# Gathering, laying out and turning the later experts' rows without TensorE, a 32-column one-hot and bf16 compares in the first routing

## The reference

```python
# 1. retention attention: q, k, v are (4, 8, 768, 64)
for t in range(S):
    state = gamma * state + outer(k[t], v[t])
    y[t] = scale * q[t] @ state
x = y.transpose(0, 2, 1, 3).reshape(3072, 512)
# 2. mixture of experts with a capacity of cap = 3072 // 8 = 384 tokens each
logits = x @ w_gate                       # (3072, 8)
for idx in np.argsort(-logits.flatten()): # best (token, expert) pairs first
    tok, e = idx // 8, idx % 8
    if assigned[tok] >= 0 or counts[e] >= cap: continue
    assigned[tok] = e; counts[e] += 1
for e in range(8):
    mask = assigned == e
    out[mask] = np.maximum(x[mask] @ w1[e], 0) @ w2[e]     # 512 -> 1024 -> 512
# 3. gated layer, 512 -> 1536 -> 512
result = (sigmoid(out @ w_gate2) * (out @ w_val)) @ w_out
```

## Time and profile before

| | |
|---|---|
| time, median of 3 runs (lowest, highest) | 1104.27 us (1103.88, 1105.41) |
| time of the profiled execution | 1104.19 us |
| its span, first to last instruction | 1102.1 us |
| PE busy | 1042.7 us, 95% of the span |
| VectorE busy | 671.9 us, 61% |
| ScalarE busy | 344.4 us, 31% |
| GpSimd busy | 133.5 us, 12% |
| DMA moved | 96.68 MB, mean 88 GB/s |
| mean granted TensorE clock | 0.976 of full speed |

### The profile page before, as it was taken

The page is one execution under the profiler, slowest core; times in us unless marked ns, Lnnn a source line. Parts: engine busy times, 40 slices in busy tenths (PEclk is TensorE's granted clock), DMA queues, the critical chain, the costliest instruction groups (busy, mean ns, idle before and its releaser), DMA issues.

```text
span 1102.1 us, 20423 instructions
## 1 busy us (share of the span) xinstructions
PE 1042.7 (95%) x7340; PEld 972.4 (88%) x7340; DVE 671.9 (61%) x1965; ACT 344.4 (31%) x659; POOL 133.5 (12%) x159
## 2 busy tenths in 40 slices
PE   6999932999999999999999999999999999999996
PEld 5888822999999999999999999999999999999995
DVE  3655568877477647765677567755776477634211
ACT  3444332332243224322432234223413241224210
POOL 5554401033010011001100110011001100110001
PEclk9999965999999999999999999999999999999998
DMA  9999443312141213211321122122312230213000
GB/s 201 250 235 245 123 134 105 114 41 69 38 125 59 58 48 107 77 48 58 105 79 48 58 90 93 39 68 78 106 39 68 67 117 20 88 50 124 8 1 29
DMA packets 172988, 96.68 MB, mean 88 GB/s; under 512 B 80224, under 2 KB 158048, under 8 KB 172896
## 3 DMA queue, kind: packets, MB, share of 16 engines
q1 hardware_dynamic: 169056, 82.92, 28.3%
q0 software_dynamic: 3840, 12.59, 3.5%
HBM read 82.90 MB, written 12.58 MB: 87 GB/s over the span
## 4 chain that ended last, share of the span: by engine, by line
PE 94%; DVE 3%; DMA 1%; issue 1%; SPq 0%; POOL 0%; ACT 0%; DVEq 0%; POOLq 0%
PE bank L1212 21%; PE bank L1214 20%; PE bank L1213 20%; PE bank L1292 6%; PE bank L1291 6%; PE bank L1290 6%; PE bank L654 2%; PE bank L631 2%; PE bank L627 2%; PE bank L589 1%; PE bank L1207 1%; PE bank L596 1%; PE bank L1172 1%; PE bank L607 1%; PE bank L641 1%; PE bank L612 1%
## 5 line engine op out<-in xcount | busy, mean ns | idle before, releaser
L1212 PE MATMUL bank<-h2h,resident 128*128 128x384 f32 x768 | 261.2, 340 | 0.0
L1214 PE MATMUL bank<-h2h,resident 128*128 128x384 f32 x768 | 257.8, 336 | 0.0
L1213 PE MATMUL bank<-h2l,resident 128*128 128x384 f32 x768 | 257.4, 335 | 0.0
L1052 DVE TENSOR_TENSOR pf<-bank,gate 128x384 f32<-128x384 f32 x96 | 53.5, 557 | 160.1 <-PE bank L1214 159.1
L1212 PEld LDWEIGHTS bank<-h2h,resident 128*128 128x128 f32 x768 | 144.3, 188 | 2.9
L1213 PEld LDWEIGHTS bank<-h2l,resident 128*128 128x128 f32 x768 | 144.3, 188 | 2.9
L1214 PEld LDWEIGHTS bank<-h2h,resident 128*128 128x128 f32 x768 | 144.1, 188 | 0.0
L781 ACT ACTIVATE ring<-ring_raw 128x512 fp32r<-128x512 f32 x192 | 117.6, 624 | 61.9 <-DMA ring_raw<-in_moe_w_out_dram 39.0
L801 ACT ACTIVATE ph<-pf 128x384 fp32r<-128x384 f32 x96 | 50.4, 525 | 263.3 <-DVE pf L1052 263.3
L1061 DVE TENSOR_TENSOR ring<-ring_raw,ring 128x512 fp32r<-128x512 f32 x192 | 126.2, 683 | 0.0
L797 ACT ACTIVATE gate<-bank 128x384 f32<-128x384 f32 x96 | 47.0, 490 | 174.9 <-PE bank L1214 174.8
(11 more groups left out here) (175 smaller groups left out, 1691.2 us busy)
## 6 DMA issues: line engine op xcount, KB each, us to landing
ring_raw<-in_moe_w_dram SPq DMA_DIRECT2D x128, 256.0 KB, 2.9
ring_raw<-in_moe_w_out_dram SPq DMA_DIRECT2D x64, 256.0 KB, 2.9
qraw<-in_q_dram SPq DMA_DIRECT2D x24, 256.0 KB, 4.4
kraw<-in_k_dram SPq DMA_DIRECT2D x24, 256.0 KB, 5.0
vraw<-in_v_dram SPq DMA_DIRECT2D x24, 256.0 KB, 5.1
xrows<-xrow SPq DMA_DIRECT2D x24, 256.0 KB, 3.8
resident_raw<-in_moe_w_gate_dram SPq DMA_DIRECT2D x12, 256.0 KB, 4.6
resident_raw<-in_moe_w_val_dram SPq DMA_DIRECT2D x12, 256.0 KB, 4.8
```

The lines of the kernel that those rows point to most:

```text
L1052: nc.vector.tensor_tensor(pf[:, f % 2, :], bank[2 * (f % 2) + 1][:, 0:CAP], gate[:, f % 2, :], ALU.mult).then_inc(p_ready, 1)
L1212: nc.tensor.matmul(ps, wh, xhi, start=start, stop=False)
L1213: nc.tensor.matmul(ps, wh, xlo, start=False, stop=False)
L1214: return nc.tensor.matmul(ps, wl, xhi, start=False, stop=stop)
```

## The change

1. **Rows.** `xrows` holds the features in another order: feature a * 128 + p stands at 4 p + a. TensorE writes the attention's rows into `ps_x` with a step of four floats.
2. **First expert.** Its 12 transposes read `xg` with a step of four floats, and go third by third: each third's four transposes wait for its own gather alone.
3. **Later experts.** TensorE doesn't turn their rows. SP stores the gathered rows to a DRAM tensor `xlaid` (`lay_rows`, one DMA of 768 KB) behind the load of weight piece 6, and reads them back by quadrants into `zg` (`quarter_rows`, four DMAs of 192 KB in pieces of 512 bytes) behind the load of piece 7. VectorE turns 32 x 32 blocks (`turn_x`, four instructions of 128 x 384) after `p_low(9)`, ScalarE takes the high part from SBUF after `p_high(9)`, VectorE the low part after `p_low(10)`. Banks 0 to 3 are no longer written at the round's end, so the next `h_tile`s wait for `gate_ready` and `p_ready` instead.
4. **One-hot.** The rank is split into its low five bits and its block of 32 (12 blocks). `make_onehot` is one instruction of 24 x 32 columns, and one more writes the ids by block; each of 24 matmuls has 32 weight columns and 24 moving columns, where there were 128 and 6. `route_ids` has four reductions, one for each quadrant. The visit stands 5 us after the one-hot's planned time where that was planned in four parts 2 us apart, so 6 planned us earlier.
5. **First routing.** `digit_f`, `prefix` and `ladder` are bf16 and the compare's innermost dimension is four units (`compare_first`), so that all its operands are bf16 and contiguous. The later routings keep the old loop order, with the bf16 operands.
6. **Last products.** `out_products(11)` issues the six matmuls on `ph` first, waiting for `ph_ready` alone, and then the three on `pl`.

The core of the diff:

```diff
...
-        part_at = [expert_at + us(1) + n * PART_GAP for n in range(PARTS)]
-        visit_at += [part_at[-1] + LATE_GAP]
+        onehot_at = expert_at + us(1)
+        visit_at += [onehot_at + LATE_GAP]
...
-                            last = nc.tensor.transpose(ps_x[:, a * P:(a + 1) * P], xTa[:, cc % 2, a, :], ident[:, :])
+                            last = nc.tensor.transpose(ps_x[:, a:DM:KD],
+                                                       xTa[:, cc % 2, a, :], ident[:, :])
...
+            def lay_rows(i):
+                sp.wait_ge(x_gathered, 16 * TT * i)
+                sp.dma_start(xlaid.rearrange("(j p) d -> p j d", p=P), xg[:, :, :]).then_inc(x_laid, 16)
+
+            def quarter_rows(i):
+                sp.wait_ge(x_laid, 16 * i)
+                for c in range(QUADS):
+                    sp.dma_start(zg[c * QUAD:(c + 1) * QUAD, :, :],
+                                 xlaid[:, c * DM // QUADS:(c + 1) * DM // QUADS].rearrange("(m p) w -> p m w", p=QUAD)).then_inc(x_quartered, 16)
                     for f in range(OUT_STREAMED):
                         sp.wait_ge(out_done, (KG - 1) * i + f + 1)
                         load_piece(f, e)
+                        if f == OUT_STREAMED - 2:
+                            lay_rows(i + 1)
+                    quarter_rows(i + 1)
...
+                else:
+                    act.wait_ge(x_turned, KD * (i - 1) + a + 1)
+                    nc.scalar.activation(xh[:, a, :], x_raw[:, a, :], ACT.Copy).then_inc(xh_ready, 1)
                     p_high(i, f)
+                    if follows and f == TURN_AT:
+                        for a in range(KD):
+                            x_high(i + 1, a)
...
+                    nc.vector.tensor_tensor(above_first[:, half * fours:(half + 1) * fours, :, :],
+                                            keys[:, tiles].rearrange("p (g t) -> p g t", t=FOLD).unsqueeze(2)
+                                            .to_broadcast([P, fours, RADIX, FOLD]),
+                                            ladder[:, :, :].unsqueeze(1).to_broadcast([P, fours, RADIX, FOLD]),
+                                            ALU.is_ge).then_inc(route_ready if half else half_compared, 1)
...
+                    link(nc.vector.tensor_copy(rank[:, :], PS_K[:, 0:U]))
+                    count_only(nc.vector.tensor_scalar(rank_block[:, :], rank[:, :], 5, None, ALU.logical_shift_right))
+                    link(nc.vector.tensor_scalar(rank_low[:, :], rank[:, :], QUAD - 1, None, ALU.bitwise_and))
+                    link(nc.vector.tensor_tensor(in_block[:, :, :], rank_block[:, :].unsqueeze(2).to_broadcast([P, U, BLOCKS]),
+                                                 block_iota[:, :].unsqueeze(1).to_broadcast([P, U, BLOCKS]), ALU.is_equal))
-                for tile in range(n * TPART, (n + 1) * TPART):
-                    last = nc.vector.tensor_scalar(onehot[:, tile, :], column[:, :], row[:, tile:tile + 1], None, ALU.is_equal)
-                last.then_inc(onehot_ready, 1)
+                nc.vector.tensor_tensor(onehot[:, :, :], column[:, :].unsqueeze(1).to_broadcast([P, U, QUAD]),
+                                                   rank_low[:, :].unsqueeze(2).to_broadcast([P, U, QUAD]), ALU.is_equal).then_inc(onehot_ready, 1)
+                nc.vector.tensor_tensor(slot_ids[:, :, :, :], in_block[:, :, :].unsqueeze(2).to_broadcast([P, U, 2, BLOCKS]),
+                                        member_id[:, :, :].unsqueeze(3).to_broadcast([P, U, 2, BLOCKS]), ALU.mult).then_inc(onehot_ready, 1)
...
+            def turn_x(i, a):
+                if a == 0:
+                    dve.wait_ge(x_quartered, 16 * QUADS * i)
+                nc.vector.transpose(x_raw[:, a, :], zg[:, :, a:DM // QUADS:KD]).then_inc(x_turned, 1)
                     prepare_next()
+                    if follows and f == TURN_AT:
+                        for a in range(KD):
+                            turn_x(i + 1, a)
+                    if follows and f == TURN_AT + 1:
+                        for a in range(KD):
+                            x_low(i + 1, a)
...
                 for j in range(TT):
+                    pe.wait_ge(third_gathered[j], 16)
+                    for a in range(KD):
+                        last = nc.tensor.transpose(bank[a][:, j * P:(j + 1) * P],
+                                                   xg[:, j, a:DM:KD], ident[:, :])
...
+                    elif g < 4:
+                        pe.wait_ge(p_ready if g % 2 else gate_ready, KG * i - 1 + g // 2)
+                    if f == KG - 1:
+                        pe.wait_ge(ph_ready, KG * i + f + 1)
+                        for j in range(TT):
+                            toks = slice(j * P, (j + 1) * P)
+                            nc.tensor.matmul(PS_OUT[j][:, :], ph[:, f % 2, toks], wh, start=False, stop=False)
+                            nc.tensor.matmul(PS_OUT[j][:, :], ph[:, f % 2, toks], wl, start=False, stop=False)
+                        pe.wait_ge(pl_ready, KG * i + f + 1)
+                        for j in range(TT):
+                            toks = slice(j * P, (j + 1) * P)
+                            nc.tensor.matmul(PS_OUT[j][:, :], pl[:, f % 2, toks], wh, start=False, stop=True).then_inc(rows_done, 1)
-                if follows:
-                    for a in range(KD):
-                        if a % 2 == 0:
-                            pe.wait_ge(gate_ready, KG * (i + 1) - 1 + a // 2)
-                        else:
-                            pe.wait_ge(p_ready, KG * (i + 1) - 1 + a // 2)
-                        transpose_x(i + 1, a)
                 out_products(KG - 1)
```

More of the change, by code:

```diff
@@ L136, in retention_moe_glu_kernel @@
         members_before = sb("members_before", [P, U], BF16)
-        past = sb("past", [P, U, TT - 1], F32)
-        thirds = sb("thirds", [P, U], F32)
-        row = sb("row", [P, U], F32)
-        slot_ids = sb("slot_ids", [P, U, TT, 2], BF16)
+        rank = sb("rank", [P, U], I32)
+        rank_low = sb("rank_low", [P, U], I32)
+        rank_block = sb("rank_block", [P, U], I32)
+        in_block = sb("in_block", [P, U, BLOCKS], BF16)
+        member_id = sb("member_id", [P, U, 2], BF16)
+        slot_ids = sb("slot_ids", [P, U, 2, BLOCKS], BF16)
         room = sb("room", [P, E], F32)
@@ L226, in retention_moe_glu_kernel @@
         ids_kept = sem("ids_kept")
+        third_gathered = [sem(f"third_gathered{j}") for j in range(TT)]
         x_gathered = sem("x_gathered")
+        x_turned = sem("x_turned")
+        x_laid = sem("x_laid")
+        x_quartered = sem("x_quartered")
         xt_done = sem("xt_done")
@@ L865, in flat, with compare_first @@
                 return ap.rearrange("p e u -> p (e u)")
+            def compare_first(keys):
+                fours = U // FOLD // 2
+                for half in range(2):
+                    tiles = slice(half * U // 2, (half + 1) * U // 2)
+                    nc.vector.tensor_tensor(above_first[:, half * fours:(half + 1) * fours, :, :],
[3 more added lines that the diff above has]
+                                            ALU.is_ge).then_inc(route_ready if half else half_compared, 1)
             def compare(keys):
@@ L929, in prepare_digits @@
                 link(nc.vector.tensor_scalar(digit_f[:, :, :], digit_i[:, :, :], 1.0, None, ALU.add))
-                compare(digit_f[:, 0, :])
+                if first:
+                    compare_first(digit_f[:, 0, :])
+                else:
+                    compare(digit_f[:, 0, :])
                 raise_by(digit_f[:, 0, :], 1)
@@ L948, in route @@
                                                         raised[:, :], ALU.mult, ALU.add))
-                    compare(prefix)
+                    if isinstance(i, int) and i == 0:
+                        compare_first(prefix)
+                    else:
+                        compare(prefix)
                     if j + 1 < DIGITS:
@@ L1023, in route_ids, with row_ids @@
                 dve.wait_ge(route_done, (i + 1) * VISITS)
[L1024 to L1026 removed]
+                sums = PS_R[0:QUAD, 0:2 * BLOCKS]
+                def row_ids(c):
+                    with nc.allow_low_precision(reason="whole numbers below N"):
+                        return nc.vector.reduce_sum(ids[c * QUAD:(c + 1) * QUAD, :],
+                                                    sums.rearrange("p (n j c) -> p c j n", n=2, c=QUADS)[:, c, :, :], AX_X)
+                for c in range(QUADS):
+                    last = row_ids(c)
+                    if c < QUADS - 1:
+                        count_only(last)
+                last.then_inc(ids_ready, 1)
                 dve.wait_ge(ids_ready, i + 1)
@@ L1083, in route_until @@
                         vis[0] += 1
-                    while vis[0] == VISITS and part[0] < PARTS and part_at[part[0]] <= at:
-                        make_onehot(part[0], i + 1)
-                        part[0] += 1
+                    if vis[0] == VISITS and not made[0] and onehot_at <= at:
```

(5 more changed lines are left out.)

139 lines of the change are left out of this document (64 added, 75 removed).

## The result

The changed kernel takes 1093.64 us (median of 4 runs, 1091.62 to 1094.14), the kernel before 1104.28 us on the same chip. The ratio is 0.9899, with a 95% interval from 0.9886 to 0.9912. A second set of four runs of the same changed kernel gave 1094.23 us (1091.56 to 1095.31). The forecast was 1091.2 us, with a range from 1088.5 to 1097.5. The median lies inside that range, and 0.14 us outside the narrower one that the forecast gave for its own case (1089 to 1093.5). The profiled execution of the changed kernel took 1091.62 us (span 1089.5), the shortest of its four. Against the profiled execution of before (1104.19 us) that is -12.6, where the sum was -13.0.

The account below looks back on a forecast made before the run. PE was taken to bound the kernel (94% of the chain), except in the first routing. Terms -2.8 - 1.5 - 0.4 - 9.2 + 0.9 = -13.0 us took 1104.2 to 1091.2 us, range 1088.5 to 1097.5.

Parts of the forecast that it names:

- its own case: The forecast of 1091.2 us holding as worked out, range 1089 to 1093.5 us, chance 0.68.
- Compares, -2.8: First routing: all-bf16 contiguous compares take 0.4 us less a pair, seven times, -2.8 us.
- An inner run of four and broadcast outer dimensions: Rival in the first routing: these keep the bf16 compare from running faster, 1094.0 us, chance 0.08.
- Ids, -1.5: First routing, rank to ids: 4.2 us for 5.7, the 24 matmuls between 0.9 and 1.4 us; -1.5 us.
- First expert's turn, -0.4: Before the first product: eight transposes done before the last third lands, bank 0 ready one transpose behind it; -0.4 us.
- Rounds, -9.2: End of seven rounds: PE's twelve transposes, 1.31 us a group, all go; one-hot matmuls' new shape costs 0; -9.2 us.
- The cover, 0: In the rounds: store, reads and VectorE's turn finish before PE wants ph(11), 1.3 us to spare; cost 0.
- The end, +0.9: Last products: first output tile complete after the seventh product instead of the third, moving the whole tail; +0.9 us.
- The strided PSUM write, 0: Attention: 96 transposes writing ps_x with a 16-byte step cost nothing more; bounds 0 and +10.5 us, taken 0.
- the first rival: Attention: the strided PSUM write slows PE, up to +10.5 us (1101.7 us); chance 0.10 for half price or more.
- the bounds of 0.56 and 1.1: VectorE's turn in the rounds: a 128 x 384 f32 block transpose takes 0.56 to 1.1 us; 1.1 taken.

Follow-up runs that it names:

- a_major: The changed kernel with the first expert's 12 transposes ordered bank by bank, waiting for each third in turn: 1091.77 us, ratio 0.9887.
- best: The changed kernel with transposes bank by bank, the old order of last products in the last round, and 48 extra matmuls before the first transposes: 1092.08 us, ratio 0.9881.
- early_turn: The changed kernel with VectorE's turn one f earlier (behind p_low(8)), the DMAs where they are: 1135.39 us, ratio 1.0269.
- warm: The changed kernel with 48 unused matmuls before the first expert's transposes, in TensorE's wait for the gather: 1091.37 us, ratio 0.988.

## Why the prediction was right

- **Compares, -2.8**: shown. A half takes 356 ns for 554, the cycle 2.40 us for 2.80, and the old order costs 2.8 back. An inner run of four and broadcast outer dimensions do not hinder it. The prediction named type and contiguity together; of the two, type alone brings nothing (555 ns).
- **Ids, -1.5**: 4.26 us for 5.71, taken at 4.2. The one-hot measured 0.96, as taken, and the 24 matmuls 0.83, just under the lower bound of 0.9.
- **First expert's turn, -0.4**: this term was mis-sized, at -0.1 (ids to first product 9.85 us for 9.93). The working had bank 0 ready "after one transpose behind" the last third. That is so only if PE has caught up by then. The thirds landed 0.6 to 0.7 us apart here, by their starts and times to landing, and four transposes at the half clock take about 1, so the last third's transposes queued behind the others, and nine of twelve ended before `xh` could start. Another order does not mend it at that clock, as `a_major` shows.
- **Rounds, -9.2**: the period gives 7 x (113.10 - 111.85) = -8.8. The turn's 1.31 us is all gone, but the new one-hot visit takes 0.70 us in the chain where it took 0.60, which the working had put at 0. The working had said that issue sets the pace of these 24 and that their new shape changes nothing; it does. These two make 1.21 of the 1.25; the rest is not placed. Had the layout with its step of four floats stayed with PE, the turn would have cost 1.45.
- **The cover, 0**: right, but partly by luck, since two errors cancel. The quarters land about 1 to 2 us later than forecast, since four issues stand in SP's queue and not one, and the turn is 1.3 us shorter. The margin is 0.8 us in round 0, where 1.3 was forecast, and 0.35 in round 1. The earlier turn shows that PE does wait once VectorE is late.
- **The end, +0.9**: +0.85, shown by undoing it.
- **The strided PSUM write, 0**: right. The 96 transposes take 274 ns, as before, and four of them 0.44 us in the chains of both kernels (101.56 us and 101.42 us on). The attention ends at 143.66 us for 143.53, and between 142.8 and 144.3 in the eleven profiles with this write, so a cost of 5 or 10 us is excluded. The rule of the Trainium skill ("SBUF — State Buffer", Door 1: The DMA port swizzle) that the first rival rested on does not hold for these transposes. Where a step of 16 bytes did cost PE something was on its reading side, 11% (1.45 us a dozen for 1.31).
- **The sum**: -2.8 - 1.5 - 0.1 - 8.8 + 0.85 = -12.35 us. Between the two profiled executions stand also the 0.9 us at the half clock that the products of before had and those of this execution had not, -0.4, and an attention 0.1 us longer: -12.65, against the -12.6 measured.
- **The median**, 1093.64, lies 2.4 us over the forecast, and the profiled execution only 0.4. That the profile agrees so well is luck in part: it was the fastest of its four. The forecast set the profiled execution of before for its median, which held there (0.08 us apart). It did not for the changed kernel: its products begin in some executions at the full clock and in others at the half, up to 2.7 us, which the working had no term for. The attention's end, which differs by over 1 us between executions, is another part. What makes the clock return sooner or later isn't settled. The Trainium skill ("TensorE: Matmul & The Clock Gate", Part 1: The HAM clock gate) says that one and the same kernel has a different number of matmuls at the lower clock from run to run; the two profiles of the changed kernel, with none and 6.0 us of them, agree. The clock's share of the 2.4 us is about 1.2, an estimate from the two kernels with extra matmuls.

## What to carry to other kernels

A wait of the bounding engine can cost more than its own length, since the engine may start again at the half clock: here waits of 3.5 to 3.7 us made rounds 5.3 to 6.6 us longer. Work moved off that engine is free only by a margin that has to be counted to its tightest round, and the count has to be made with the data's landing and the operation's time apart, since errors in the two can hide each other. When a gather is used in pieces as they land, compare the spacing of the landings with the time that each piece's work takes. Here that work was the slower of the two, the last piece queued behind it, and turning the order round gained only 0.1 to 0.2 us.

## What the runs showed of the hardware

- A block transpose of 128 x 384 f32 with an input step of 16 bytes takes VectorE 0.84 us (28 of them, 0.82 to 0.87), between the bounds of 0.56 and 1.1.
- PE's f32 transposes cost nothing more when they write PSUM with a step of 16 bytes (274 ns each, 0.44 us for four in the chain), and 1.45 for 1.31 us a dozen when they read SBUF with one.
- The clock fell from 1.00 to 0.50 during an idle stretch of PE of 3.33 us (`best`) and during or right behind waits of 3.5 to 3.7 us (`early_turn`), and stayed at 1.00 through one of 2.49 us (`warm`).
- A store of 768 KB landed in 4.5 us, where 256 KB had taken 3.8.
- In the three kernels of the changed layout with extra matmuls, the first transpose started 6.6 to 6.9 us after the first gather went out, in the others 5.0 to 6.2. In the one with 88 of them PE was busy with these until then. One profile of each; whether the matmuls have to do with it was not tried, and the kernel before shows no such difference (6.42 and 6.38).
